# A router's lanes and counts moved to VectorE, between the scans of a causal attention

## What is computed

```python
scores = scale * np.matmul(q, k.transpose(0, 1, 3, 2))      # causal, softmax over keys
local = np.matmul(softmax(scores), v)
mem_out = (phi(q) @ M_prev) / (phi(q) @ z_prev + 1e-6)
x = g * mem_out + (1 - g) * local                             # g = sigmoid(beta), per head
logits = x @ w_gate
e_idx = np.argmax(logits, axis=1)
for e in range(E):                                            # one expert for each token
    mask = e_idx == e
    h = np.maximum(x[mask] @ w1[e], 0.0)
    out[mask] = gate_w[mask, None] * eom[mask, e, None] * (h @ w2[e])
```

## Time and profile before

| | |
|---|---|
| median of 3 runs | 464.05 us (464.01 to 465.46) |
| the profiled execution | 464.11 us, its span 462.2 us |
| TensorE busy | 453.9 us, 98% of the span |
| VectorE busy | 303.8 us, 66% |
| ScalarE busy | 276.9 us, 60% |
| GpSimd busy | 195.3 us, 42% |
| granted clock of TensorE, mean | 0.998 of full speed |

### The profile page before, as it was taken

One profiled execution on the slowest core, in us unless ns is written; L12 is line 12 of the kernel. 1 busy time (PEld: TensorE's weight loads), 2 busy tenths in 40 slices (PEclk: granted clock), 3 DMA queues, 4 the chain that ended last, 5 costly groups with the idle time before them and its releaser, 6 DMA issues.

```text
span 462.2 us, 11671 instructions
## 1 busy us (share of the span) xinstructions
PE 453.9 (98%) x4252; PEld 355.9 (77%) x4252; DVE 303.8 (66%) x780; ACT 276.9 (60%) x622; POOL 195.3 (42%) x192
## 2 busy tenths in 40 slices
PE   8999999999999999999999999999999999999995
PEld 6677777677777777787888888888888888888884
DVE  4889898989999997877222399222237957952220
ACT  5889988999999875344222577222237837832221
POOL 7567776769889846251222111221111312221111
PEclk9999999999999999999999999999999999999999
DMA  7234433567544723647322279410117966600000
GB/s 232 83 113 143 134 105 106 191 200 221 194 119 143 239 58 98 210 124 272 129 69 69 72 242 342 171 38 13 46 48 236 326 238 193 223 1 23 23 24 37
DMA packets 44883, 64.09 MB, mean 139 GB/s; under 512 B 7198, under 2 KB 26142, under 8 KB 44832
## 3 DMA queue, kind: packets, MB, share of 16 engines
q1 hardware_dynamic: 40672, 53.81, 35.2%
q0 software_dynamic: 4160, 9.60, 6.5%
HBM read 56.77 MB, written 10.90 MB: 146 GB/s over the span
## 4 chain that ended last, share of the span: by engine, by line
PE 97%; ACT 1%; issue 1%; DVE 0%; another core or an unknown queue 0%; POOL 0%; ACTq 0%; POOLq 0%; DVEq 0%
PE S L1469 23%; PE S L1652 19%; PE S L1653 18%; PE S L1654 18%; PE STK L1469 4%; PE TP_ps L1469 4%; PE TP_ps L1465 3%; PE TP_ps L1692 2%; PE STK L1465 2%; PE STK L1687 2%; PE S L1465 1%; ACT w_hi0b L778 0%; PE TP_ps L1675 0%; DVE probs L970 0%
## 5 line engine op out<-in xcount | busy, mean ns | idle before, releaser
L749 ACT ACTIVATE probs<-probs,neg_max 128x128 f32<-128x128 f32 (+2 forms) x144 | 82.8, 582 | 5.1 <-DVE neg_max L970 4.5
L695 POOL DMA_INDIRECT out<-x_ring,slot_tok_i x23 | 26.9, 1171 | 134.9 <-ACT x_ring L835 102.9
L1652 PE MATMUL S<-w_hi,x_hi 128*128 128x512 f32 x180 | 70.2, 390 | 0.0
L1654 PE MATMUL S<-w_hi,x_lo 128*128 128x512 f32 x180 | 70.1, 389 | 0.0
L1653 PE MATMUL S<-w_lo,x_hi 128*128 128x512 f32 x180 | 70.0, 389 | 0.0
L618 POOL DMA_INDIRECT x_ring<-x_tokens,slot_tok_i x29 | 32.0, 1105 | 85.2 <-DMA out<-x_ring,slot_tok_i 67.9
L1469 PE MATMUL S<-k_pair,q_pair 64*128 64x256 f32 (+5 forms) x384 | 64.3, 442 | 0.0
L1652 PE MATMUL S<-w_hi0b,hid_hi 128*128 128x512 f32 x152 | 61.7, 406 | 0.0
L970 DVE CUSTOM_DVE_ANT_0 probs<-S,mask 128x128 f32<-128x128 f32 (+3 forms) x128 | 55.1, 487 | 6.8 <-PE S L1469 6.3
L1653 PE MATMUL S<-w_lo0b,hid_hi 128*128 128x512 f32 x152 | 59.4, 391 | 0.0
L1654 PE MATMUL S<-w_hi0b,hid_lo 128*128 128x512 f32 x152 | 59.2, 389 | 0.0
(11 more groups left out here) (230 smaller groups left out, 875.9 us busy)
## 6 DMA issues: line engine op xcount, KB each, us to landing
w_raw<-in_moe_w SPq DMA_DIRECT2D x60, 512.0 KB, 5.3
q_pair<-in_qt SPq DMA_DIRECT2D x15, 288.0 KB, 2.9
k_pair<-in_kt SPq DMA_DIRECT2D x15, 288.0 KB, 3.4
v_nat<-in_v SPq DMA_DIRECT2D x16, 256.0 KB, 3.5
x_tokens<-x_out SPq DMA_DIRECT2D x16, 256.0 KB, 2.4
x_ring<-in_moe_w SPq DMA_DIRECT2D x2, 512.0 KB, 4.9
m_aug<-in_m_aug SPq DMA_DIRECT2D x1, 648.0 KB, 6.6
m_turned<-in_m_t SPq DMA_DIRECT2D x1, 512.0 KB, 3.6
```

Of the source, the lines that this page charges most:

```text
L695: nc.gpsimd.indirect_dma_start(out=out[:, :], out_offset=bass.IndirectOffsetOnAxis(ap=slot_tok_i[:, t:t + 1], axis=0), in_=x_ring[:, t % X ...
L749: last = nc.scalar.activation(pr, pr, ACT.Exp, bias=neg_max[:, slot, h:h + 1], scale=-1.0, accum_out=sums[g % 2][:, at, 0:1])
L1652: T.matmul(dst, hi, part(i, k)[:, cols], start=first, stop=False)
L1654: return T.matmul(dst, lo, part(i, k)[:, cols], start=False, stop=last)
```

## The change

The five lanes of batch 0 and of batch 1, ten operations, leave GpSimd, where they stood in pairs 13 and 14, and go to VectorE in pairs 9 to 15. A new function `routing_between`, called behind `read_loc` and ahead of the scans of slots 3 to 6, takes two counts (`so_far(1, 1)` from pair 8 to pair 10, `so_far(2, 3)` from pair 13 to pair 14) and three of the lanes. `order_rest` moves from pair 12 to pair 8, and `place(2)` from behind pair 14's tail scan to ahead of pair 15's. The semaphore `placed` is dropped; instead each `place` ends in a link.

```diff
-            def lanes(b):
-
-                pool.wait_ge(r_consts_dve, 1)
-                pool.wait_ge(placed, b + 1)
-                for t in range(b * TPB, (b + 1) * TPB):
-                    nc.gpsimd.tensor_scalar(r_lanes[:, t, :], iota_f[:, :], r_lane[:, t:t + 1], None, ALU.is_equal).then_inc(lanes_done, 1)
...
-                elif 0 <= g - 9 - KD < 2:
-                    lanes(g - 9 - KD)
...
-                lane = V.scalar_tensor_tensor(r_lane[:, ts], r_tile_of[:, ts, E], -float(P), r_slot[:, ts], ALU.mult, ALU.add)
-                if b < 2:
-                    lane.then_inc(placed, 1)
-                else:
-                    link(lane)
+                link(V.scalar_tensor_tensor(r_lane[:, ts], r_tile_of[:, ts, E], -float(P), r_slot[:, ts], ALU.mult, ALU.add))
...
+            def routing_between(g):
+                if g == 10:
+                    so_far(1, 1)
+                elif g == 13:
+                    lanes(1, 0, 2)
+                elif g == 14:
+                    so_far(2, 3).then_inc(hot_done, 1)
+                elif g == 15:
+                    lanes(1, 4, 5)
...
                 elif g == 8:
                     turns()
-                    so_far(1, 1)
+                    order_rest()
                 elif g == 9:
                     place(0)
+                    lanes(0, 0, 2)
                 elif g == 10:
                     largest(1)
                     choose(1)
+                    lanes(0, 2, 3)
                 elif g == 11:
                     open_gate(1)
                     so_far(1, 2)
+                    lanes(0, 3, 5)
                 elif g == 12:
                     place(1)
-                    order_rest()
                 elif g == 13:
                     largest(2)
+                    lanes(1, 2, 4)
                 elif g == 14:
                     scale(0, LAST)
                 elif g == 15:
+                    place(2)
                     early_tiles()
                     lanes(2, 0, 3)
...
                 elif g == 13:
                     choose(2)
-                    so_far(2, 3).then_inc(hot_done, 1)
                     open_gate(2)
                 elif g == 14:
                     read_ranks(2)
-                    place(2)
                 elif g == 15:
                     lanes(2, 3)
...
                 if valid(x):
                     read_loc(x)
+                if valid(g):
+                    routing_between(g)
```

More of the change, by code:

```diff
@@ L277, in memory_attention_top1_moe @@
     scale_stored = [sem(f"scale_stored{n}") for n in range(2)]
-    placed = sem("placed")
     lanes_done = sem("lanes_done")
```

## The result

The changed kernel takes 467.62 us (median of 6 runs, 466.74 to 468.91), the kernel before 463.81 us (6 runs beside them). The ratio is 1.0087, with a 95% interval of 1.0067 to 1.0106: slower by 0.9%, 3.8 us, where I had forecast 465.0. The size is that of my second rival, 467.4.

A forecast was written before the change was run, and what follows sets the result against it. TensorE, busy 98% of the span, was taken as the bound. Terms +0.84, −0.11, −0.04, then −0.35 in pair 15 and +0.67 at the table gave +1.0 us on 464.05: forecast 465.0, range 463.7 to 466.0.

The forecast's parts named there:

- rival 2: Lanes on VectorE are held beside GpSimd, in pairs 9, 13 and 15: +3.4 us, 467.4; chance 0.12.
- pair 10, scan at L10 + 3.53: First 384-wide scan 3.53 us after pair 10's first turn_w load, behind two lanes and a count: +0.84 us.
- pairs 11 and 12: Added lanes in pair 11 hidden by slack, order_rest's move to pair 8 hidden too: both 0.
- pair 13, two lanes in the slack ahead of the scan: Two lanes (0.39) between read_loc and scan nearly fit 0.37 of spare time: loss 0.02 instead of 0.13, −0.11 us.
- pair 14, the cast held beside `phi_T`: Earlier copy gains, but the count's cast waits for GpSimd: loss 0.83, −0.04 us (to −0.49 with a free cast).
- pair 15 and the table, load at L15 + 10.70: Pair 15's scan on time, −0.35; table's first load 10.70 us after its first turn_w load, +0.67.
- the price of a lane: Each further lane on VectorE takes 0.195 us, from three taking 0.67 and two 0.48.
- `place(2)`: Moved ahead of pair 15's tail scan, takes 0.84 on the path; idle before the table's load grows by 0.67.
- pair 9's second lane: Under rival 2, this lane falls into the last part of GpSimd's q_pos: +0.37 us.

The follow-up runs named there:

- e3: Changed kernel with place(2) moved back behind pair 14's tail scan; 467.06 us, ratio 1.0070 to the kernel before.
- p1: Kernel before plus two scratch lanes between read_loc and the slot-3 scan in pairs 4 to 7; 469.71 us, ratio 1.0128.
- p3: Kernel before plus two scratch comparisons against a constant between read_loc and the slot-3 scan in pairs 4 to 7; 469.19 us, ratio 1.0112.
- e1: Changed kernel with the three lanes of pairs 13 and 15 moved behind the scans; 465.97 us, ratio 1.0042 to the kernel before.
- e6: Kernel before with only place(2) moved from behind pair 14's tail scan to pair 15's routing place; 463.75 us, ratio 1.0005.
- e5: Kernel before with only so_far(1,1) moved from pair 8 to pair 10, between read_loc and the scan; 463.89 us, ratio 1.0005.
- e4: Changed kernel with the lanes of batches 0 and 1 back on GpSimd; 465.31 us, ratio 1.0031 to the kernel before.
- f1: Changed kernel with VectorE's lanes in the form that also sums its output (accum_out), casts unchanged; 466.91 us, ratio 1.0074 to the kernel before.
- f2: Changed kernel with accumulating lanes and running counts reduced straight into bf16, without the cast; 465.78 us, ratio 1.0053 to the kernel before.
- p5: Kernel before plus one scratch lane between read_loc and the slot-3 scan in pairs 4 to 7; 468.75 us, ratio 1.0103.
- p7: Kernel before plus two scratch operations with two SBUF inputs between read_loc and the slot-3 scan in pairs 4 to 7; 469.34 us, ratio 1.0125.

## Why the prediction was wrong, by its own steps

The times come from two places: what a step is forecast to do between L10 and the table, and what the trace shows there. From L10 to the table I had +1.0; it became +3.71.

| step of the prediction | forecast us | measured us |
|---|---|---|
| pair 10, scan at L10 + 3.53 | +0.84 | +1.45, scan at L10 + 4.18 (with the cast free in e3: +0.84, L10 + 3.55) |
| pairs 11 and 12 | 0 | 0.00 and 0.00 |
| pair 13, two lanes in the slack ahead of the scan | −0.11 | +1.18, scan at L13 + 4.00 |
| pair 14, the cast held beside `phi_T` | −0.04 | −0.09, scan at L14 + 3.46 (forecast 3.48) |
| pair 15 and the table, load at L15 + 10.70 | +0.32 | +1.17, load at L15 + 11.55 |

**The step that failed** is the price of a lane: "A lane on VectorE: three take 0.67 and two 0.48, so each further one takes 0.195", used in pair 13 as "0.37 against 0.39, loss 0.02" and in pair 15 as "the single lane ahead of the scan (0.195) fits into 0.37". That price is right where GpSimd isn't at work (pair 13 of the changed kernel, ahead of the tail scan: two lanes in 0.48) and even beside the middle of `q_pos` (pair 11: two in 0.47), and wrong beside `phi_T`, where the first lane takes the rest of GpSimd's operation and the second the whole of the next. These two misses are 1.29 and 0.85 of the 2.70 that are missing in the sum; pair 10 is another 0.61, and pair 14 came 0.05 better than forecast. In pair 10 I had priced the lanes ahead of it at 0.39, where the first alone was held to 0.80, and the count's cast as free: it came 3.82 us after L10, behind `phi_T`, and was held by the next operation, `logits_h`, with which my sum didn't reckon.

What led to it was the argument against rival 2, that a lane of 128 numbers takes longer than the 128-wide cast "so the lane looks like an operation that runs at single rate and differently from those held". p1 and p3 show the lane held all the same, so what its length seemed to say of its rate was no guide. I had the row that would have been the better guide: `r_part`, of the same kind as the lane, held beside `w_lo`, and I priced the cast by it and not the lane.

**Rival 2** had the mechanism, the places and the sum (+3.4). In its terms, each counted over the forecast, pair 13 was to cost +1.10 (+1.29 measured; it had the scan at L13 + 3.77 and took the second lane as free), pair 15 +0.93, where e1 shows 0.85 for the lane, and pair 9's second lane +0.37 (0.39 between the changed kernel and e3). What it didn't have is that the 0.39 carries the cast of pair 10 from the end of `phi_T` into `logits_h`.

**Right** were: that pair 10 is the worst place for new work, the held cast of pair 14 and with it the missing gain there, the free pairs 11 and 12 (`order_rest` in pair 8 costs nothing, and its 0.55 is no loss), and `place(2)`: 0.67 forecast, 0.68 between the changed kernel and e3; 0.32 forecast for the whole of pair 15 without a held lane, 0.31 in e6. The terms of the count and of the place, taken alone in e5 and e6, were 0.74 and 0.31 in the traces, and not to be seen in the times. That pair 10 came to +0.84 in e3, as forecast for its lanes and its count together, is in part luck: the count's cast ran free there, and was held in the changed kernel, e1, e4, e5 and f1.

**Open** stays who decides in pair 9 whether the lanes or `q_pos` wait: the two traces agree to 0.01 us in when both ask. And the changed kernel's executions spread from 466.74 to 468.91, of which pair 10's two outcomes (0.61) and the late copy of `out_T` (0.8) can explain a part; I have one trace of it and can't say what the slowest hold.

## What to carry to other kernels

Before work moves to VectorE, look at what GpSimd does at that moment, not at how long the work is: beside a GpSimd operation with two inputs (here `phi_T`, `w_lo`, `lg_new`) a plain compare, a cast or a compare with two inputs from SBUF cost what was left of it (here up to 1.3 us for 0.2 us of work), and a chain of two met the next one too. Beside one with a single input (`q_pos`) it depended on the moment. Put such steps where GpSimd idles, or choose a form that isn't held; here reductions, the compare with an accumulator, and the scans that read PSUM ran through. And price an operation by the row of its own kind under the same neighbour, even where its tile and its length are quite different.

## What the runs showed of the hardware that I had not expected

- The length of an operation gave no sign of whether it would be held: lanes that follow one another after 0.195 us, no faster than reductions of the same length (0.20), were held to 1.32 us, and the compare with an accumulator, 0.265 apart, was never held. Which mode a lane runs in no run shows.
- Beside `q_pos` (1.64 us) lanes and casts that asked 0.57 to 0.87 us after its start took their plain 0.28 and 0.17; `r_tile_of`, at 0.1, took 0.60, and lanes that asked at 1.06 and 1.26 lasted until its end.
- It may go both ways: in e3 the first lane ran free beside `q_pos`, which took 1.74 us instead of 1.64. One trace has this.
- More GpSimd work ahead of `phi_T` moves the holding, too. In e4, with ten lanes back on GpSimd, `phi_T` of pair 14 began 2.56 us after L14 and not 2.11, the cast (asked at L14 + 3.32, in the changed kernel at L14 + 2.98) was held until its end, and pair 14 took 11.89 instead of 11.45.
- TensorE's clock fell after short idling in one trace, and in another it didn't. After 1.3 us of idling in 5, f2's granted clock was 0.50 for 2 us and 0.77 and 0.94 around them; f1, which idled as much (3.68 busy of 5) in its profiled execution, kept 1.00 there, but its executions lie at 464.7 with a mean clock of 0.999 or more and at 466.8 to 469.9 with 0.996 or less. The changed kernel's profiled execution idled 0.96 of the 5 us ahead of the table, with 1.00. So a wait of TensorE can cost more than itself, in f2 1.58 us, but what tips it no run here shows.
- The clock also fell at the start of the span: in the profiled executions of e3, p5 and p7 the granted clock was 0.50 from 14 to 16 us. L10 came at 109.95 in e3 and, less the 3.4 and 5.8 of their scratch work, at 110.0 in p5 and 110.2 in p7, where before and the changed kernel have 107.07 and 106.54. So parts of a kernel are to be compared from a landmark, not from the start of the span.
